# A new table of ticks for the attention stages, loads, weight units and filler products of an attention + two-MoE kernel

## The reference

```python
B, H, S, D = 2, 8, 576, 64 ; factor = 4
q_d, k_d, v_d = (x.reshape(B, H, S // 4, 4, D).mean(axis=3) for x in (q, k, v))
out_up    = repeat(softmax(q_d k_d^T / 8) v_d, 4, axis=2)
out_local = softmax(where(|i - j| < 4, q k^T / 8, -1e9)) v
x = (out_up + out_local) as (B * S, H * D) = (1152, 512)

h = x @ w_in1                       # 512 -> 2048
P = a0 + a1 h + a2 h^2 + a3 h^3 ;  Q = 1 + |b0||h| + |b1| h^2
x = (P / (Q + 1e-6)) @ w_out1       # 2048 -> 512

h = x @ w_in2
out = (h * tanh(softplus(h))) @ w_out2
```

## Time and profile before

| | us |
|---|---|
| median of 3 runs | 471.25 (469.7 to 475.39) |
| the profiled execution, its own time | 470.82 |
| its span, first to last instruction | 469.0 |
| PE busy in the span | 454.7 |
| start of `hidden(0)` | 41.44 |
| start of `output_first(0)` | 60.36 |

### The profile page before, as it was taken

One profiled execution on the slowest core, in us unless ns is written; L12 is line 12 of the kernel. 1 busy time (PEld: TensorE's weight loads), 2 busy tenths in 40 slices (PEclk: granted clock), 3 DMA queues, 4 the chain that ended last, 5 costly groups with the idle time before them and its releaser, 6 DMA issues.

```text
span 469.0 us, 10932 instructions
## 1 busy us (share of the span) xinstructions
PE 454.7 (97%) x4312; PEld 332.8 (71%) x4312; DVE 388.4 (83%) x658; ACT 306.2 (65%) x565; POOL 210.0 (45%) x228
## 2 busy tenths in 40 slices
PE   6997999999999999999999999999999999999997
PEld 5776878887888889899999975444445555557663
DVE  5777799999769787676879988889999888878894
ACT  4568798988657784778777777654745555554543
POOL 3878549874625313111227547258652222212122
PEclk9999899999999999999999999999999999999999
DMA  7998647323123000020011411112100200000101
GB/s 134 168 283 247 145 95 195 93 66 74 34 63 80 1 3 3 1 91 1 3 46 25 157 46 50 41 46 95 40 1 0 92 0 2 0 1 1 67 3 45
DMA packets 46544, 29.80 MB, mean 64 GB/s; under 512 B 31900, under 2 KB 40092, under 8 KB 46492
## 3 DMA queue, kind: packets, MB, share of 16 engines
q1 hardware_dynamic: 44972, 28.57, 23.1%
q10 hardware_dynamic: 1520, 0.53, 0.5%
HBM read 26.73 MB, written 2.36 MB: 62 GB/s over the span
## 4 chain that ended last, share of the span: by engine, by line
PE 86%; POOL 6%; DMA 3%; ACT 2%; SPq 1%; issue 1%; DVE 0%; ACTq 0%; POOLq 0%
PE bank L629 38%; PE bank L673 20%; PE bank L653 19%; PE bank L592 3%; DMA work<-in_moe_w_out 2%; POOL w L1103 1%; DMA late<-in_v 1%; PE bank L497 1%; POOL work L1101 1%; POOL g_l L1115 1%; PE bank L515 1%; PE bank L578 1%; POOL late L1103 1%; PE bank L533 1%; POOL late L1067 1%
## 5 line engine op out<-in xcount | busy, mean ns | idle before, releaser
L1115 POOL TENSOR_TENSOR g_l<-work,g_h 128x512 f16<-128x512 f32 (+2 forms) x81 | 88.4, 1092 | 224.2 <-ACT g_h L804 203.3
L629 PE MATMUL bank<-x_h,w 128*128 128x256 f16 (+1 forms) x640 | 102.3, 264 | 1.7 <-DVE x_l L941 1.6
L653 PE MATMUL bank<-g_h,w 128*128 128x256 f16 (+1 forms) x640 | 101.3, 262 | 0.6 <-POOL g_l L1115 0.6
L629 PE MATMUL bank<-x_h,late 128*128 128x512 f16 (+2 forms) x384 | 96.9, 326 | 0.0
L794 ACT ACTIVATE bank<-work,coef 128x512 f32<-128x512 f32 (+2 forms) x81 | 52.4, 647 | 66.9 <-DVE work L971 64.0
L673 PE MATMUL bank<-late,g_h 128*128 128x512 f16 x288 | 92.0, 379 | 0.0
L629 PE MATMUL bank<-x_l,w 128*128 128x256 f16 (+1 forms) x320 | 84.4, 264 | 0.0
L653 PE MATMUL bank<-g_l,w 128*128 128x256 f16 (+1 forms) x320 | 83.8, 262 | 0.0
L653 PEld LDWEIGHTS bank<-g_h,w 128*128 128x128 f16 x640 | 60.9, 98 | 8.6 <-issue 2.8
L629 PEld LDWEIGHTS bank<-x_h,w 128*128 128x128 f16 x640 | 61.3, 98 | 7.5 <-issue 1.9
L629 PE MATMUL bank<-x_l,late 128*128 128x512 f16 (+2 forms) x192 | 62.6, 326 | 0.0
(11 more groups left out here) (103 smaller groups left out, 776.9 us busy)
## 6 DMA issues: line engine op xcount, KB each, us to landing
raw<-in_moe_w_in SPq DMA_DIRECT2D x10, 512.0 KB, 4.5
raw<-in_moe_w_out SPq DMA_DIRECT2D x10, 512.0 KB, 4.0
late<-in_k SPq DMA_DIRECT2D x16, 144.0 KB, 3.9
late<-in_v SPq DMA_DIRECT2D x8, 288.0 KB
late<-in_moe_w_out SPq DMA_DIRECT2D x4, 512.0 KB, 4.3
late<-in_moe_w_in SPq DMA_DIRECT2D x4, 512.0 KB, 4.1
out<-w SPq DMA_DIRECT2D x8, 256.0 KB, 2.5
late<-in_v SPq DMA_DIRECT2D x15, 97.5 KB
```

What stands on the lines that cost most here:

```text
L629: last = pe.matmul(ps, w_in(l, wp)[:, kk, at], x[:, kk, t0:t0 + n], start=(kk == 0 and wp == 0 and x is x_h), stop=(kk == KD - 1 and wp == 1))
L653: last = pe.matmul(ps, w_out(0, wp)[:, f, 128 * d:128 * (d + 1)], g[q % 4][:, i * n:(i + 1) * n], start=False, stop=(f == FT - 1 and d % 2 ...
L1115: pool.tensor_tensor(g_l[q % 4][:, 0:w], num[q % 4][:, 0:w], g_h[q % 4][:, 0:w], ALU.subtract).then_inc(g_rest, 1)
```

## The change

All numbers of STAGES and UNITS are replaced, TWO_BANKS goes from 37.7816 to 38.2847, and the filler counts change. The code, the engine of each stage, the instructions in each, LAYERS and the tiles of the layers stay. UNITS changes no unit's engine. From the diff:

```diff
-    TWO_BANKS = 37.7816
+    TWO_BANKS = 38.2847
-    FILLER = {"turn_k": 8, "turn_p": 7, "turn_d": 2, "out_down": 1, "score_down": 1, "score_local": 3, "out_local": 3}
+    FILLER = {"turn_k": 4, "turn_p": 7, "turn_d": 5, "out_down": 7, "score_down": 2, "score_local": 4, "turn_q": 1, "turn_p_end": 1}
...
-              ("pe", "turn_d", (29.032, 32.032, 39.302, 44.531, 60.0, 65.062, 80.062, 86.275)),
+              ("pe", "turn_d", (20.535, 26.785, 35.535, 41.96, 57.975, 68.958, 74.969, 85.4)),
...
-             (3, 21.032, 16.282, 22.282, 1),
+             (3, 5.785, 35.035, 15.785, 1),
```

More of the change, by code:

```diff
@@ L80, in attention_moe_moe @@
     LAYERS, PREFILL, SLOT = 39.125, 4.25, 2.5
-    TWO_BANKS = 37.7816
+    TWO_BANKS = 38.2847
     ACT_PARTS, DVE_PARTS, POOL_PART = (0.2, 0.3, 0.6), (0.56, 0.93, 1), 1.25
-    FILLER = {"turn_k": 8, "turn_p": 7, "turn_d": 2, "out_down": 1, "score_down": 1, "score_local": 3, "out_local": 3}
+    FILLER = {"turn_k": 4, "turn_p": 7, "turn_d": 5, "out_down": 7, "score_down": 2, "score_local": 4, "turn_q": 1, "turn_p_end": 1}
     FIRST_FILLER = 1
[L85 to L105, removed]
[4 rows of a table removed]
-              ("dve", "join", (27.532, 37.032, 42.693, 47.862, 68.708, 71.875, 88.05, 92.562)),
[3 rows of a table removed]
-              ("act", "x_head", (31.532, 33.782, 44.712, 47.975, 71.25, 73.287, 88.542, 92.975)),
-              ("dve", "x_rest", (34.282, 38.229, 47.325, 51.75, 71.0, 73.708, 89.375, 94.375))]
@@ new lines, in attention_moe_moe @@
+    UNITS = [(0, 0.785, 24.035, 29.285, 0),
+             (2, 2.535, 25.285, 33.285, 0),
+             (4, 4.535, 26.285, 33.035, 0),
+             (6, 0.285, 23.535, 35.285, 0),
+             (1, 2.785, 27.035, 12.535, 1),
+             (8, 5.535, 34.785, 41.666, 0),
+             (3, 5.785, 35.035, 15.785, 1),
+             (10, 6.535, 37.035, 43.475, 0),
+             (5, 6.785, 37.285, 30.285, 1),
+             (12, 6.285, 36.785, 41.738, 0),
+             (7, 10.035, 46.708, 46.958, 1),
+             (14, 9.535, 44.933, 47.042, 0),
+             (9, 9.785, 44.802, 46.208, 1),
+             (11, 15.535, 52.975, 54.375, 0),
+             (13, 13.535, 51.542, 51.958, 1),
+             (15, 16.535, 57.0, 56.75, 1),
+             (16, 29.035, 91.958, 90.588, 1),
+             (17, 33.785, 112.2, 136.875, 1),
+             (18, 32.035, 117.2, 131.875, 0),
+             (19, 18.535, 101.125, 101.875, 0),
+             (20, 31.535, 97.325, 111.875, 0),
+             (21, 38.705, 144.375, 147.975, 1),
+             (22, 36.285, 141.5, 145.475, 0),
+             (23, 37.785, 137.2, 140.787, 1),
+             (24, 152.9, 149.7, 151.875, 0),
+             (25, 201.875, 156.875, 155.475, 1),
+             (26, 102.562, 153.05, 157.975, 0),
+             (27, 161.125, 149.375, 163.625, 1),
+             (28, 174.825, 154.7, 160.475, 1),
+             (29, 210.475, 166.125, 172.562, 0),
+             (30, 215.062, 167.975, 169.458, 0),
+             (31, 216.875, 169.292, 173.625, 1)]
```

58 lines of the change are left out of this document (27 added, 31 removed), and 9 rows, old and new, of the table STAGES.

## The result

The changed kernel takes 476.24 us (median of 20 runs, 473.78 to 479.34) beside 471.28 us for the kernel before (median of 20, 468.81 to 475.50): a ratio of 1.0098, 95% interval 1.0075 to 1.0121. It is slower by 1%, less than the 2% that tell a change here, but clearly not level. The forecast was 470.0, and its range ended at 475.5. The profiled execution of the changed kernel has a span of 474.5 us, 5.5 more than before.

A forecast was written before the change was run, and what follows sets the result against it. PE was taken as the bound nearly everywhere (busy 454.7 of 469.0 us). Gains of 0.5 us up to the first output and 0.5 behind it gave a 468.0 span, 469.8 profiled, 470.0 us predicted; range 466.0 to 475.5.

The forecast's parts named there:

- What bounds it: Whole kernel: PE is the bound nearly everywhere; a table can change the first 60 us and stalls of half a microsecond.
- The way to turn_p(0): Prologue: turn_p(0) starts at 24.3 us instead of 21.02, 3.3 us later, behind POOL's pool_q(2) and norm_local(0).
- hidden(0): First hidden tile on PE: starts at 44.6 us, 3.2 later than before, a loss of 1.0 us after work already done.
- The first read of hidden(0): ACT's first read of the first hidden tile, released by POOL's weight rests: near 49.4 us, before 48.91.
- The loads are hidden: Weight loads come 10 us or more before their tiles; SP's new waits precede windows needed tens of microseconds later.
- ACT reaches unit 1's head near 37: ACT ahead of POOL's weight rests: unit 1's head is there at 38 us, its rest ends at about 43.
- The first rival: Weight rests arrive late, units 8 and 3 loaded behind load_v(3): +3 to +5 us, 473 to 475; chance 0.27.
- From the read to the output: ACT's first read to first output: 11.4 us to POOL's rest of g at 60.8; output at 61.3, gain 0.5.
- the slow tile is not paid: Hidden tiles before the first output: the 1.3 us of one low-clock tile falls away, PE having no comparably empty stretch.
- Behind it: From the first output to the end: PE's list otherwise the same, some POOL stalls go; -0.5 us in all.
- The sum: Whole kernel: 469.0 - 0.5 - 0.5 = 468.0 us span, 469.8 profiled, 470.0 predicted.
- The rival of the clock: Longer PE idle gaps in the prologue lower the clock, 1.3 us per hidden tile: 471 to 474; chance 0.08.

The follow-up runs named there:

- all three edits: Changed kernel with load_v(0..3) and load_windows(2) moved ahead in SP's queue and unit 3's rest moved from POOL to DVE: 472.97 us, ratio 1.0025.
- all three with POOL's list later: Changed kernel with all three edits, plus pool_v(4), pool_v(5) and unit 9's rest one tile later each on POOL: 472.51 us, ratio 1.0027.

## Why the prediction was wrong

**What bounds it: right.** PE is busy for 96% of the span, and in the profiled execution the loss lies ahead of the first output.

**The way to turn_p(0): right.** Forecast 24.3, measured 23.75, released by POOL's L1085 as forecast.

**hidden(0): too early by 2.7 us.** Forecast 44.6, measured 47.28, and now it is PE's list that sets it, with 0.23 us of waiting. From `turn_p(0)` on that list was put at 19.7 us, and takes 23.3 (23.75 to 47.05). The step that failed is that it took over the stalls of the kernel before less one, at the full clock. New are a wait of 1.33 us of `out_down(0)` for ACT (28.68 above), one of 0.77 ahead of `out_down(1)`, and the lower level from 34 to 37, where 3.00 us of PE at 0.50 are worth 1.5: 3.6 in all. The late v loads are not in it: with them early, H0 is still at 46.87. Nor is it a matter of one execution: in all kernels with the changed order H0 lies between 45.6 and 47.9. No experiment changed PE's order by itself.

**The first read of hidden(0): too early by 4.4 us.** Forecast 49.4, measured 53.81. The rests of units 1 and 3 were to begin at 38, and began at 41.36: 3.4 of the 4.4 us. Two steps failed there.

The first is the sentence "The loads are hidden". I looked at the weight loads and at the heads on ACT, and not at the v loads, which the change moves past two q loads and a weight unit in SP's queue. POOL waits 2.56 us for `load_v(1)`; `load_v(3)` waits in turn for `pool_v(1)`, takes 8.03 us from issue to use, and POOL's list comes to unit 1 only at 41.36. The second is "ACT reaches unit 1's head near 37". The head, right behind that of unit 4, was written at 40.68:

```profile
39.64 1.04 ACT L763 ACTIVATE w<-work 128x1024 f16<-128x1024 f32 x1
```

Ahead of it `put_p(2)` waits 1.43 us for PE's `turn_p(2)`, which is late with PE's list, and unit 4's head 0.65 us for its transfer. So without the late v loads POOL could have begun 0.7 us earlier, and in the run with early v loads it began at 40.20, 1.2 us earlier, waiting for ACT. The v loads are one to one and a half of the 4.4 us in the traces; the other 2.7 of the late start are ACT's head. The last 0.9 is the length of the rests: 12.3 us in place of the 11.4 that 38 to 49.4 stands for.

The first rival named just this link (`load_v(3)` behind `pool_v(1)`), with the right sign and a chance of 0.27; 473 to 475 was its price, and 476.2 was measured. It should have been the forecast. Its other half, the late head of unit 3, did not matter: that head is done at 44.9, and POOL comes to unit 3 at 48.13.

**From the read to the output: 13.8 us, forecast 11.4 on POOL's side, and 15.3 from hidden(0) on PE's.** Two terms failed, and both come out at the same time. On POOL the 11.4 of before was carried over, though `sum_local(3)` now stands behind DVE's first piece of tile 0, so that POOL idles until 56.58 and then has 9.8 us of norms, unit 5's rest and `pool_v(4)` in a row up to the rest of g at 66.37. On PE, `out_local(2)` waits twice (1.06 and 0.81), and `hidden(2)` starts 0.62 late and runs at the lower level, 57.88 to 62.17 in place of 2.62 us. The sentence "the slow tile is not paid" is wrong: it is paid at the same tile as before, and PE was busy for 7.51 us of the 10 from 50 to 60, as empty as the stretch that I named.

**Behind it: forecast -0.5, measured -0.3.** From O0 to the end the changed kernel takes 406.9 us, before 408.6, and 1.4 of the difference is the attention work done earlier. The number is right by chance: one output tile near 181 runs at the lower level,

```profile
181.07 4.26 PE bank L653 x24
```

1.6 us more than 2.62. In the kernel with all three edits this tile takes 2.73, and the stretch from O0 to the end 405.2 us. The same tile takes 4.39 us in two more profiled executions (v loads and windows early; all three with POOL's list later). Without it the new order behind the first output is worth some 2 us. This is from single executions and was not tested by itself.

**The sum** is then: forecast 468.0 for the span; +2.7 at `hidden(0)`, +3.6 from there to the output (20.3 in place of 16.7), +0.2 behind it: 474.5. (Added up as written, the forecast's own terms give 61.4 for the output and 470.2 for the time, 0.1 and 0.2 more than it states. That changes nothing.)

**The rival of the clock: small.** The mean granted clock over the 20 executions of the changed kernel is 0.987, and over the 28 to 33 of the kernel before that ran beside each set of experiments 0.989 to 0.990. Among those of before, time and clock go together, 2.3 to 2.8 us for 0.01. By that the clock is worth 0.5 to 0.8 us of the 5, an estimate. At an equal mean clock of 0.99, straight lines through the executions give 475.5 us for the changed kernel, 471.7 for the one before, and 473.2 with all three edits. So most of the loss, and most of what the edits give back, is not the clock.

What is open: the three edits together give back 0.73 of the 0.98 points, and the rest, 0.25, has an interval that reaches to nothing. How the 0.73 is made up of the chain's pieces is read from single executions. The late H0, which all kernels with the changed order have, was not tested. Where in the prologue the clock falls differs from kernel to kernel (34 to 37 us in the changed one, 16 to 27 with all three edits, where H0 is at 46.84 all the same), and no run here holds it fixed.

## What to carry to other kernels

Follow every transfer that a table moves, the small ones of a late stage too: a load is hidden only if the engine that reads it has other work in front of the place where it lands, and an in-order queue that waits for that engine passes the delay on (here `load_v(1)` to `pool_v(1)` to `load_v(3)` to the weight rests). Where two engines end a stage at the same time, easing one shows nothing until the other is eased too; moving work from one to the other needs a look at what that one does in that microsecond. Take the places of two or three executions before reading a shift of a microsecond: here kernels with the same order up to a point reached it up to 2.3 us apart. And when a rival names a concrete chain and the forecast has only "hidden" against it, work out the chain before giving chances.

## What the runs showed of the hardware

A piece of a weight rest on POOL (L1101, L1103) takes 0.62 and 1.15 us while DVE is idle, and up to 1.59 and 2.01 us while DVE runs its own rests. In the changed kernel the first six pieces, from 41.36 to 51.8, are long, and the last two short; DVE's last rest of the stretch:

```profile
49.16 1.62 DVE L947 SCALAR_TENSOR_TENSOR w<-raw,w 128x1024 f16<-128x1024 f32 x1
```

ends at 50.8, and DVE then waits until 55.0. Eight pieces at the short times would be 7.1 us, and they take 12.3. The Trainium skill (SBUF — State Buffer, Who interferes with whom) says that a VectorE instruction with two SBUF inputs and a GpSimd instruction that reads SBUF exclude each other, and that the later one waits. The traces agree, and both orders stand in the kernel before:

```profile
38.04 1.16 POOL L1103 TENSOR_TENSOR w<-work,w 128x512 f16<-128x512 f32 x1
38.12 2.15 DVE L947 SCALAR_TENSOR_TENSOR w<-raw,w 128x1024 f16<-128x1024 f32 x1
46.53 1.17 DVE L947 SCALAR_TENSOR_TENSOR w<-raw,w 128x1024 f16<-128x1024 f32 x1
```

Where POOL starts first, at 38.04, it takes its short time and DVE's rest, begun 0.08 us later, takes 2.15. Where DVE starts first, at 46.53, it takes 1.17, and POOL's piece at 46.71 takes 2.01. So over a stretch both sides lengthen. DVE's first x_l (L941) takes 1.80 us in the changed kernel, beside POOL's norms, and 0.68 with the v loads early, while POOL is idle. The forecast had POOL's durations in the earlier trace rows, and priced them as spread, not as an effect of DVE's five weight rests beside them.

The lower clock level (1.2 GHz) came in three profiled executions at one and the same output tile, near 181, with PE busy for 10.00 of 10 us from 170 to 180 and the clock at 1.00 there. An idle gap is not what went ahead of it. What did, in all three, is an `out_local` (80 small products, 2.45 us). In the changed kernel the two other stretches at the lower level come behind an `out_local` too (31.02 to 33.07, and 53.75 to 57.26 with two waits). The kernel with all three edits has the same 2.45 us at 175.48 and no lower level behind them, so this alone does not decide it, and no run here tells what does.

A v load of 288 KB took 8.03 us from its issue at 28.61, between three weight units issued from 26.32 to 28.97, and 5.49 us from 20.69, between two issued at 20.03 and 21.20. The weight units, of 512 KB, took 5.1 us in the median over the whole kernel, and 5.9 to 8.4 in the groups issued between 15 and 35 us. In that stretch the DMA engines are busy for nine tenths of the time.
